# Branch order and one-by-one turns in a fused attention, router and gated-product kernel

## The chip, the cores and the metric

The kernel runs on one core of a Trainium2 chip. The metric is the device time of one execution in microseconds. The core's engines run their own instruction streams and meet through semaphores: TensorE (PE, matrix products and transposes), VectorE (DVE), ScalarE (ACT), GpSimd (POOL) and SyncE (SP, which here only issues transfers).

## The reference

Three stages, each feeding the next, all in float32:

```
scores = q k^T / sqrt(64)                  # batch 2, 8 heads, 768 positions, head size 64
keep = (key < n_sink) | (0 <= query - key < window)      # n_sink 4, window 128
x = softmax(where(keep, scores, -1e9)) v   # laid out as 1536 tokens x 512

P = exp(x w_gate - max)                    # 1536 x 8 experts, then 8 rounds of row and column scaling
y = sum over e of P[:, e] * relu(x w1[e]) w2[e]          # 512 -> 1024 -> 512, 8 experts

out = ((y w_a) * (y w_b)) w_out            # 512 -> 1536 -> 512
```

`n_sink` and `window` are inputs, so the program must also be right for other values.

## The kernel before, in words

Every float32 operand is split into a high part, which is what TensorE's reduced float32 format keeps, and a low part, the rest. A product is made of three passes: high by high, high by low, low by high. ScalarE makes high parts (a copy that rounds), VectorE makes low parts (original minus high part).

**Two ways through attention.** VectorE reads the two sizes and writes a flag, `in_range`, at the start. Each engine loads it (`chosen`, line 205) and branches. With `fits == 1` (at most 16 sinks, window at most 129) a fast path runs that computes only the needed band of the scores, for pairs of heads, with `LEAD = 2` pairs in flight. With `fits == 0` a general path runs, written with loops. With the inputs here the fast path is taken. GpSimd and TensorE have the code of the general path ahead of that of the fast path, as two Ifs after each other (TensorE: `pe.If(fits == 0)` at line 730, then `pe.If(fits == 1)`). SP, ScalarE and VectorE have an If for the fast path and an Else for the general one, so there the fast path's code stands first and a branch at its end (lines 348, 1080, 1472) passes over the general path. What follows is common to both.

VectorE's fast path starts with `in_window` (lines 1283, 1285), the low parts of queries and keys of pair 0 (`split_pair_lo`, lines 1307, 1310), `make_mask` (1291, 1294) and `mask_scores` (1321). TensorE's scores of pair 0 (line 562) wait for these low parts. At the end of attention VectorE copies the router's logits (`logits_out`, line 1419) and splits the first expert's weights (line 1385), for whose second half GpSimd forms sums (lines 430 to 435) and ScalarE high parts (line 988).

**Experts.** A product of two 2 x 2 blocked matrices is done with seven block products, P1 to P7, instead of eight. Each is six matmuls of 128 x 384 (lines 655 to 657). `sub` 0 and 1 are the two halves of the hidden columns, `pi` 0 and 1 the two batches of tokens. Sums and differences of blocks that the method needs are made by GpSimd, ScalarE (`keep`) and VectorE (`add`).

**The hand-over to the last stage.** The sum over experts (`acc`) is in token order and must be turned so that the model dimension lies on partitions. `turn_sums(v)`, v = 0 to 23, does one piece: two or four transposes on TensorE (line 726) into one PSUM bank. `x2_hi(v)` (line 1140) takes the high part on ScalarE and `x2_lo(v)` (line 1625) the low part on VectorE. Turns 0 to 11 are for batch 0, 12 to 23 for batch 1. The pieces of batch 1 alternate between two PSUM banks: turn v waits for low part v - 2. Turns 12 to 23 stand between the products of the last stage's first group (k = 0), which uses batch 0 only. The tables `LEAD_TURNS` and `FIRST_TURNS` say behind which product each turn stands. The first product of the second group (P1, k = 1, sub 0) waits until all 24 low parts exist.

The order on each engine is the order in which the code is written. On ScalarE and VectorE the parts stand between the copies and additions of group k = 0: `keep_a`, `keep_b` (ScalarE, lines 1186, 1190), `add_a`, `add_b` (VectorE, lines 1714, 1721), `gated` (VectorE, lines 1729, 1733: product of the two factors), `gated_hi` (ScalarE, 1197), `gated_lo` (VectorE, 1741), and `wo_hi`, `wo_lo`, the parts of the output weights (1202, 1747).

Of the kernel before, what the change touches and what calls it, by code (L numbers as in the profile page):

```python
# [33 lines left out]
def build(nc, qT, kT, v, sizes, w_gate, w1, w2, w_a, w_b, w_out, out):  # L34
    B, H, D, S = qT.shape
# [5 lines left out]
    KC = DM // P  # L41
# [14 lines left out]
    LEAD = 2  # L56
    RING = 4
    PAIRS = HEADS // 2
# [19 lines left out]
    with ctx:  # L78
# [95 lines left out]
        s = {n: sem(n) for n in names}  # L174
# [118 lines left out]
        def _(sp):  # L293
# [10 lines left out]
            def load_values(b):  # L304

                sp.dma_start(vs[:, b], v_rows[b][:, :, 0:P]).then_inc(s[f"v_in{b}"], 16)
                sp.wait_ge(s["sink_zero"], 1)
                sp.dma_start(vz[0:SINK, b], v_rows[b][0:SINK, 0, 0:P]).then_inc(s[f"v_in{b}"], 16)

            def load_w1(e, hf, sub):  # L310
                f0 = hf * FM * P + sub * SUBF
                sp.dma_start(raw1[:, sub], w1_rows[:, bass.ds(e * KC, KC), f0:f0 + SUBF])\
                    .then_inc(s[f"raw1_in{sub}"], 16)
# [31 lines left out]
            load_values(0)  # L345
            sp.dma_start(wg[:], w_gate.rearrange("(c p) e -> p c e", p=P)).then_inc(s["gate_in"], 16)
            fits = chosen(sp)
            with sp.If(fits == 1):
                load_values(1)
                for sub in range(2):  # L350
                    load_w1(0, 0, sub)
                for i in range(1, KC):
                    for b in range(B):
                        load_pair(i, b)
                sp.wait_ge(s["qk_lo"], 2 * PAIRS)
                load_w2(0, 0)
            with sp.Else():
                for landed in ("qk_in0", "qk_in1"):
                    sp.wait_ge(s[landed], 32)
                sp.wait_ge(s["v_in0"], 32)  # L360
                for sub in range(2):
                    load_w1(0, 0, sub)
                with sp.Fori(0, QT) as j:
                    with sp.Fori(0, KC) as c:
                        for b in range(B):
                            general_loads(j, c, b)
                sp.wait_ge(s["d_lo"], 2 * GROUPS + 2)
                load_w2(0, 0)
            load_step(0, 1)
            with sp.Fori(1, E) as e:  # L370
# [172 lines left out]
        def _(pe):  # L543
# [385 lines left out]
                        mm.then_inc(s["z_ps"], 1)  # L929

            FULL = ("P1", "P5", "P2", "P6", "P3", "P7")
            LEAD_TURNS = {"P1": (12,), "P5": (13,), "P2": (14,), "P6": (15, 16), "P3": (17,), "P7": (18,)}
            FIRST_TURNS = {"P1": (19,), "P5": (20,), "P2": (21,), "P6": (22, 23)}
            for name in FULL:
                gated_product(name, 0, 0)
                for v in LEAD_TURNS[name]:
                    turn_sums(v)
            for k in range(KT):
                for name in FULL:
                    gated_product(name, 1, k)  # L940
                    if k == 0:
                        for v in FIRST_TURNS.get(name, ()):
                            turn_sums(v)
                    if k == 0 and name == "P1":
                        gated_product("P4", 0, 0)
                if k + 1 < KT:
                    gated_product("P1", 0, k + 1)
                    gated_product("P4", 1, k)
                    for name in FULL[1:]:
                        gated_product(name, 0, k + 1)  # L950
                    project2(k, 0)
                    gated_product("P4", 0, k + 1)
                    for tt in range(1, HTILES):
                        project2(k, tt)
# [8 lines left out]
        def _(act):  # L963
# [113 lines left out]
                                     accum_out=esum[:, 0, 0:1]).then_inc(s["d_exped"], 1)  # L1077

            fits = chosen(act)
            with act.If(fits == 1):  # L1080
                for p in range(LEAD):
                    split_pair_hi(p)
                for p in range(-LEAD, PAIRS):
                    if p == -1:
                        gate_parts_hi()
                    pair(p)
            with act.Else():
                with act.Fori(0, QT) as j:
                    with act.Fori(0, KC) as c:
                        for b in range(B):  # L1090
                            for a in range(2):
                                general_head(j, c, b, a)
                act.wait_ge(s["d_t"], 1)
                nc.scalar.copy(xoh_op[:, 4, :], x32_op[:, 5, :]).then_inc(s["d_thi"], 1)
                act.wait_ge(s["d_t"], 5)
                nc.scalar.copy(xoh_op[:, 0:2, :], x32_op[:, 0:2, :])
                nc.scalar.copy(xoh_op[:, 3, :], x32_op[:, 3, :])
                nc.scalar.copy(xoh_op[:, 2, 0:BEFORE_LAST], x32_op[:, 2, 0:BEFORE_LAST])
                nc.scalar.copy(xoh_op[:, 5:7, 0:BEFORE_LAST], x32_op[:, 5:7, 0:BEFORE_LAST])\
                    .then_inc(s["d_thi"], 1)  # L1100
                act.sem_inc(s["t_hi"], 10)
                gate_parts_hi()
                ws_hi(0, 0, (0, 1, 2))

            def gate_exp():

# [100 lines left out]
            x2_hi(13)  # L1207
            x2_hi(14)
            keep_a("P6", 0, 1)
            for v in (15, 16, 17, 18):  # L1210
                x2_hi(v)
            for k in range(KT):
                first = k == 0
                keep_b("P1", k, 0)
                if first:
                    x2_hi(19)
                    keep_a("P4", 0, 3)
                keep_b("P5", k, 2)
                if first:
                    x2_hi(20)  # L1220
                    x2_hi(21)
                keep_b("P6", k, 1)
                if first:
                    x2_hi(22)
                    x2_hi(23)
                    wo_hi(0)
                gated_hi(k, 0)
                gated_hi(k, 1)
                if k + 1 < KT:
                    keep_a("P1", k + 1, 0)  # L1230
# [17 lines left out]
        def _(dve):  # L1248
# [220 lines left out]
                nc.vector.tensor_copy(x32_flat[rows, bass.ds(at, P)], ps[rows, O_BANK, 0:P]).then_inc(s["d_lo"], 1)  # L1469

            fits = chosen(dve)
            with dve.If(fits == 1):
                in_window()
                split_pair_lo(0)
                make_mask()
                mask_scores(0, (0, 1))
                split_pair_lo(1)
                for p in range(-LEAD, PAIRS):
                    if p == -1:
                        gate_parts_lo()  # L1480
                    pair(p)
            with dve.Else():
                dve.wait_ge(s["d_pos"], 2)
                for jh in range(2):
                    with dve.Fori(0, QT // 2) as j3:
# [31 lines left out]
                dve.sem_inc(s["x_ready"], 1)  # L1517
                gate_parts_lo()
                ws_lo(0, 0, (0, 1, 2))


            links = 0
# [240 lines left out]
            x2_lo(12)  # L1763
            x2_lo(13)
            add_a(0, 0)
            for v in (14, 15, 16):
                x2_lo(v)
            add_a(0, 1)
            x2_lo(17)
            add_a(0, 2)  # L1770
            for v in (18, 19, 20):
                x2_lo(v)
            for k in range(KT):
                t = k // B
                add_b(k, 0)
                if k == 0:
                    x2_lo(21)
                gated(k, 0)
                if k > 0:
                    gated_lo(k, 0)  # L1780
                if k == 0:
                    x2_lo(22)
                    x2_lo(23)
                add_b(k, 1)
                add_b(k, 2)
                gated(k, 1)
                gated(k, 2)
                if k == 0:
                    wo_lo(0)
# [56 lines left out]
```

## Time and profile before

| | |
|---|---|
| time, median of 3 runs | 1434.7 us (1434.7 to 1436.05) |
| profiled execution | 1434.7 us, its span 1432.9 us |
| TensorE busy | 1399.3 us, 98% of the span |
| VectorE, ScalarE, GpSimd busy | 55%, 35%, 14% |
| matmuls | 7592 |
| mean granted TensorE clock | 0.999 of full speed |

Times inside the execution are counted from the start of the span. Attention with its pairs ends at about 126 us, the experts at about 1149 us, the last stage fills the rest. In the answers, a name such as `ps<-xoh,wsh` reads: written tile, then the tiles read. `xoh`, `xol` are high and low parts of the tokens, `wsh`, `wsl` those of weights, `pr` the masked scores, `pt` the turned probabilities (early on also the mask's raw material), `st` and `ab` staged block products, `hh` and `hl` parts of the hidden values. A time in brackets at a row's end is how long the engine was idle before the row, and whose instruction ended that.

### The profile page before, as it was taken

Reading aid. Unit: us, or ns where it says so; the run is one execution under the profiler, and the core shown is the slowest. Engines: PE = TensorE matmul, PEld = TensorE weight load, DVE = VectorE, ACT = ScalarE, POOL = GpSimd, SP = SyncE. Lnnn points to the kernel's source line nnn. Section 1 sums busy time; section 2 is a strip of 40 time slices with the busy share of each in tenths; the row PEclk is TensorE's granted clock in tenths of the full one; section 3 lists DMA queues with packets and bytes.
Section 4 is the critical chain, followed back from the end, with each engine's and each line's share of the span. In section 5 each row is a group of like instructions: output and inputs, shape, how many; then the busy total and the mean of one; then the engine's idle time right before and its main releaser. Section 6 shows DMA issues by size and latency. Waiting matters only on the chain.

```text
span 1432.9 us, 21020 instructions
## 1 busy us (share of the span) xinstructions
PE 1399.3 (98%) x7592; PEld 1255.9 (88%) x7592; DVE 788.4 (55%) x1507; ACT 497.7 (35%) x1081; POOL 207.2 (14%) x263
## 2 busy tenths in 40 slices
PE   5988999999999999999999999999999999999999
PEld 4777889888899988889998888999888999999998
DVE  6887665544445454444545444454544566656665
ACT  5885132322223232222323222242322343232331
POOL 1256010101101010110101011010101321111100
PEclk9999999999999999999999999999999999999999
DMA  4221000101000010100001010000101001101002
GB/s 149 94 87 31 30 30 30 40 22 58 31 29 29 29 37 23 57 29 29 29 29 41 21 55 29 29 29 29 44 22 38 16 31 44 30 31 45 30 1 88
DMA packets 49726, 56.48 MB, mean 39 GB/s; under 512 B 2432, under 2 KB 37376, under 8 KB 49664
## 3 DMA queue, kind: packets, MB, share of 16 engines
q1 hardware_dynamic: 44768, 53.26, 11.5%
q10 hardware_dynamic: 4896, 2.41, 0.6%
q8 instruction: 38, 0.62, 0.2%
q14 instruction: 24, 0.20, 0.0%
HBM read 52.51 MB, written 3.15 MB: 39 GB/s over the span
## 4 chain that ended last, share of the span: by engine, by line
PE 91%; DVE 4%; ACT 4%; issue 1%; POOL 0%; DMA 0%; DVEq 0%; POOLq 0%
PE ps L655 29%; PE ps L657 29%; PE ps L656 29%; ACT pr L1007 2%; ACT pt L1016 1%; PE ps L726 1%; PE ps L585 1%; PE ps L562 0%; DVE wide L1349 0%; DVE wsl L1385 0%; DVE pr L1321 0%; DVE acc L1760 0%; DVE x L1353 0%; DVE w2l L1310 0%; PE ps L681 0%
## 5 line engine op out<-in xcount | busy, mean ns | idle before, releaser
L655 PE MATMUL ps<-xoh,wsh 128*128 128x384 f32 x1232 | 414.3, 336 | 3.0 <-ACT st L1122 3.0
L657 PE MATMUL ps<-xol,wsh 128*128 128x384 f32 x1232 | 413.2, 335 | 0.0
L656 PE MATMUL ps<-xoh,wsl 128*128 128x384 f32 x1232 | 412.7, 335 | 0.0
L655 PE MATMUL ps<-w2h,hh 128*128 128x512 f32 x912 | 360.7, 396 | 0.8 <-DVE acc L1603 0.8
L657 PE MATMUL ps<-w2l,hh 128*128 128x512 f32 x912 | 359.8, 395 | 0.0
L656 PE MATMUL ps<-w2h,hl 128*128 128x512 f32 x912 | 359.6, 394 | 0.0
L1608 DVE SCALAR_TENSOR_TENSOR acc<-ps,g_now,acc 128x512 f32<-128x512 f32 x180 | 135.1, 751 | 201.6 <-PE ps L657 201.6
L655 PEld LDWEIGHTS ps<-xoh,wsh 128*128 128x128 f32 x1232 | 231.9, 188 | 7.1 <-ACT st L1122 3.3
L656 PEld LDWEIGHTS ps<-xoh,wsl 128*128 128x128 f32 x1232 | 231.9, 188 | 3.7
L657 PEld LDWEIGHTS ps<-xol,wsh 128*128 128x128 f32 x1232 | 231.6, 188 | 0.0
L657 PEld LDWEIGHTS ps<-w2l,hh 128*128 128x128 f32 x912 | 171.7, 188 | 39.8
L655 PEld LDWEIGHTS ps<-w2h,hh 128*128 128x128 f32 x912 | 171.9, 188 | 37.0 <-DVE acc L1603 1.2
L656 PEld LDWEIGHTS ps<-w2h,hl 128*128 128x128 f32 x912 | 171.8, 188 | 35.7
L430 POOL TENSOR_TENSOR sst<-raw 128x256 f32<-128x256 f32 x44 | 32.9, 749 | 1029.5 <-DVE wsl L1385 1029.5
L1122 ACT COPY st<-ps 128x384 f32<-128x384 f32 x96 | 46.0, 480 | 374.3 <-PE ps L657 374.3
L1581 DVE TENSOR_TENSOR st<-ps,st 128x384 f32<-128x384 f32 x96 | 53.5, 558 | 124.1 <-PE ps L657 124.1
L1581 DVE TENSOR_TENSOR ab<-ps,ab 128x384 f32<-128x384 f32 x96 | 53.5, 558 | 85.7 <-PE ps L657 85.7
L1589 DVE SCALAR_TENSOR_TENSOR hl<-ps,hh 128x384 fp32r<-128x384 f32 x64 | 35.7, 558 | 77.4 <-ACT hh L1135 76.7
L988 ACT CAST wsh<-raw 128x512 fp32r<-128x512 f32 x88 | 52.1, 621 | 58.2 <-POOL raw L432 58.2
L1385 DVE TENSOR_TENSOR wsl<-raw,wsh 128x512 fp32r<-128x512 f32 x88 | 62.3, 722 | 17.9 <-ACT wsh L988 17.9
L1135 ACT ACTIVATE hh<-ps 128x384 fp32r<-128x384 f32 x64 | 31.5, 493 | 106.1 <-PE ps L657 106.1
L1122 ACT COPY ab<-ps 128x384 f32<-128x384 f32 x96 | 46.1, 480 | 55.5 <-PE ps L657 55.5
(148 smaller groups left out, 1308.5 us busy)
## 6 DMA issues: line engine op xcount, KB each, us to landing
raw<-in_w_dram SPq DMA_DIRECT2D x32, 512.0 KB, 3.5
raw<-in_w_dram SPq DMA_DIRECT2D x16, 1024.0 KB, 5.1
rk<-in_k_dram SPq DMA_DIRECT2D x8, 384.0 KB, 3.7
rq<-in_q_dram SPq DMA_DIRECT2D x8, 384.0 KB, 4.2
raw<-in_w_a_dram SPq DMA_DIRECT2D x6, 512.0 KB, 3.6
raw<-in_w_b_dram SPq DMA_DIRECT2D x6, 512.0 KB, 3.5
raw<-in_w_out_dram SPq DMA_DIRECT2D x6, 512.0 KB, 3.6
out_dram<-acc SPq DMA_DIRECT2D x12, 256.0 KB, 2.0
```

What stands on the lines that cost most here:

```text
L430: nc.gpsimd.tensor_tensor(s1, a21, a22, ALU.add).then_inc(s["s_sum"], 1)
L655: nc.tensor.matmul(o, ah, bh, start=first, stop=False, skip_group_check=True)
L656: nc.tensor.matmul(o, al, bh, start=False, stop=False, skip_group_check=True)
L657: return nc.tensor.matmul(o, ah, bl, start=False, stop=last, skip_group_check=True)
L988: nc.scalar.copy(ws_piece(wsh, sub, j), ws_raw(sub, j)).then_inc(s["w_hi"], 1)
L1007: nc.scalar.activation(t, t, ACT.Exp, bias=nmin[:, r, j:j + 1], scale=-1.0, accum_out=esum[:, r, j:j + 1]).then_inc(s["exped"], 1)
L1122: nc.scalar.copy((st, ab)[sub][:, slot, :], ps[:, bank_of(sub, name), 0:HT]).then_inc(s["kept"], 1)
L1135: nc.scalar.activation(hh[:, 2 * sub + 1, 0, :], ps[:, bank_of(sub, "P4"), 0:HT], ACT.Relu)\
L1385: nc.vector.tensor_tensor(ws_piece(wsl, sub, j), ws_raw(sub, j), ws_piece(wsh, sub, j).bitcast(F32), ALU.subtract)\
L1581: nc.vector.tensor_tensor(t, ps[:, bank_of(sub, name), 0:HT], t, ALU.add).then_inc(s["c_add"], 1)
L1589: nc.vector.scalar_tensor_tensor(out=hl[:, 2 * sub + m, half, :], in0=src, scalar=0.0, in1=hh[:, 2 * sub + m, half, :].bitcast(F32), op0=A ...
L1608: ins = nc.vector.scalar_tensor_tensor(out=acc[:, tile, :], in0=ps[:, Y_BANK + k % 2, :], scalar=g_now[:, tile:tile + 1], in1=acc[:, tile, ...
```

## The change

Three engines (SP, ScalarE, VectorE) get the layout that TensorE and GpSimd have: the general path's code first, under `If(fits == 0)`, then the fast path's under `If(fits == 1)`. The statements in each path are the same. And the 12 turns of batch 1 are spread one behind each product: 12 to 17 behind the six products of sub 0, 18 to 23 behind the six of sub 1, instead of by the two tables, with ScalarE's and VectorE's orders adapted.

```diff
@@ SP, and in the same way ScalarE (line 1080) and VectorE (line 1472)
             fits = chosen(sp)
-            with sp.If(fits == 1):
-                load_values(1)
-                for sub in range(2):
-                    load_w1(0, 0, sub)
...
-            with sp.Else():
+            with sp.If(fits == 0):
                 for landed in ("qk_in0", "qk_in1"):
                     sp.wait_ge(s[landed], 32)
...
                 sp.wait_ge(s["d_lo"], 2 * GROUPS + 2)
+                load_w2(0, 0)
+
+            with sp.If(fits == 1):
+                load_values(1)
+                for sub in range(2):
+                    load_w1(0, 0, sub)
...
@@ TensorE
-            LEAD_TURNS = {"P1": (12,), "P5": (13,), "P2": (14,), "P6": (15, 16), "P3": (17,), "P7": (18,)}
-            FIRST_TURNS = {"P1": (19,), "P5": (20,), "P2": (21,), "P6": (22, 23)}
-            for name in FULL:
+            for x, name in enumerate(FULL):
                 gated_product(name, 0, 0)
-                for v in LEAD_TURNS[name]:
-                    turn_sums(v)
+                turn_sums(12 + x)
             for k in range(KT):
-                for name in FULL:
+                for x, name in enumerate(FULL):
                     gated_product(name, 1, k)
                     if k == 0:
-                        for v in FIRST_TURNS.get(name, ()):
-                            turn_sums(v)
-                    if k == 0 and name == "P1":
+                        turn_sums(18 + x)
+                    if k == 0 and x == 0:
                         gated_product("P4", 0, 0)
@@ ScalarE
-            for v in (15, 16, 17, 18):
+            for v in (15, 16, 17):
                 x2_hi(v)
...
                 if first:
-                    x2_hi(19)
+                    x2_hi(18)
                     keep_a("P4", 0, 3)
                 keep_b("P5", k, 2)
                 if first:
+                    x2_hi(19)
                     x2_hi(20)
+                keep_b("P6", k, 1)
+                if first:
                     x2_hi(21)
-                keep_b("P6", k, 1)
+                    wo_hi(0)
+                gated_hi(k, 0)
                 if first:
                     x2_hi(22)
                     x2_hi(23)
-                    wo_hi(0)
-                gated_hi(k, 0)
                 gated_hi(k, 1)
@@ VectorE
-            for v in (14, 15, 16):
-                x2_lo(v)
+            x2_lo(14)
+            x2_lo(15)
             add_a(0, 1)
-            x2_lo(17)
+            x2_lo(16)
             add_a(0, 2)
-            for v in (18, 19, 20):
+            for v in (17, 18, 19, 20):
                 x2_lo(v)
...
                 add_b(k, 0)
-                if k == 0:
-                    x2_lo(21)
                 gated(k, 0)
...
                 if k == 0:
+                    x2_lo(21)
                     x2_lo(22)
+                add_b(k, 1)
+                gated(k, 1)
+                if k == 0:
                     x2_lo(23)
-                add_b(k, 1)
                 add_b(k, 2)
-                gated(k, 1)
                 gated(k, 2)
```

**VectorE behind the test of the flag.** Before, the rows behind the test are those of the fast path:

```order
L205 TENSOR_LOAD in_range
L205 ISA x2
L1472 COMPARE_AND_BRANCH
L1283 TENSOR_SCALAR pt<-pt,lim 128x672
L1285 SCALAR_TENSOR_TENSOR pt<-pt 128x672
L1307 TENSOR_TENSOR wsl<-rq,wsh 128x768
```

After, the general path stands behind the test, and the fast path 280 rows further on; this is where the two meet (L1511 is the second If's test):

```order
L1385 TENSOR_TENSOR wsl<-raw,wsh 128x512 x2
L1385 TENSOR_TENSOR wsl<-sst,wsh 128x768
L1472 UNCONDITIONAL_BRANCH
L1511 COMPARE_AND_BRANCH
L1283 TENSOR_SCALAR pt<-pt,lim 128x672
L1285 SCALAR_TENSOR_TENSOR pt<-pt 128x672
```

The branch over the general path has moved from the end of the fast path to its start.

**VectorE at the end of the fast path.** Before, what stands behind the last sums of attention is a branch and the general path:

```order
L1364 TENSOR_TENSOR x<-x 128x384
L1367 TENSOR_TENSOR x<-x 128x384
L1369 TENSOR_TENSOR x<-x 128x384
L1472 UNCONDITIONAL_BRANCH
L1485 UNCONDITIONAL_BRANCH
```

After, it is the common part (L1419 copies the logits):

```order
L1364 TENSOR_TENSOR x<-x 128x384
L1367 TENSOR_TENSOR x<-x 128x384
L1369 TENSOR_TENSOR x<-x 128x384
L1511 UNCONDITIONAL_BRANCH
L1419 COPY lt<-ps 40x384 x2
```

Nothing stands between the two parts any more but a branch to the next instruction.

**VectorE at the last turns.** L1625 (L1626 after) are the low parts, `st<-ps,st` is `add_b`, `st<-st,ab` is `gated`, `w2l<-raw,w2h` are the output weights. Before:

```order
L1721 TENSOR_TENSOR st<-ps,st 128x384
L1625 TENSOR_TENSOR xol<-ps,xoh 128x2x128
L1729 TENSOR_TENSOR st<-st,ab 128x384
L1625 TENSOR_TENSOR xol<-ps,xoh 128x4x128 x2
L1721 TENSOR_TENSOR st<-ps,st 128x384 x2
L1729 TENSOR_TENSOR st<-st,ab 128x384 x2
L1747 TENSOR_TENSOR w2l<-raw,w2h 128x512 x2
```

After:

```order
L1722 TENSOR_TENSOR st<-ps,st 128x384
L1730 TENSOR_TENSOR st<-st,ab 128x384
L1626 TENSOR_TENSOR xol<-ps,xoh 128x2x128
L1626 TENSOR_TENSOR xol<-ps,xoh 128x4x128
L1722 TENSOR_TENSOR st<-ps,st 128x384
L1730 TENSOR_TENSOR st<-st,ab 128x384
L1626 TENSOR_TENSOR xol<-ps,xoh 128x4x128
L1722 TENSOR_TENSOR st<-ps,st 128x384
L1730 TENSOR_TENSOR st<-st,ab 128x384
L1748 TENSOR_TENSOR w2l<-raw,w2h 128x512 x2
```

The last low part now has an addition and a product between it and the one before it. On TensorE turn 23 (four transposes) stands behind P7, directly ahead of the second group's first product, where before turns 22 and 23 stood together behind P6. On ScalarE the two casts of the output weights and the first gated cast now stand ahead of the last two high parts.

## Rows read from the trace of the kernel before

**Rows 1.** The page, chain that ended last: shares of the span by engine.
```profile
PE 91%; DVE 4%; ACT 4%; issue 1%; POOL 0%; DMA 0%; DVEq 0%; POOLq 0%
```

**Rows 2.** Branch instructions by line: ns min/median/max, first and last start in us.
```profile
L730 PEldq COMPARE_BRANCH  x1: 5486/5486/5486, 5.9 to 5.9; - x1
...
L1472 DVEq COMPARE_BRANCH x2: 50/56/63, 5.8 to 125.4; - x2
```

**Rows 3.** Chain of waits, 4 to 14 us: start, us, what.
```profile
5.94 0.58 DVE pt L1283
...
9.23 2.51 issue
11.74 1.71 PE ps L562 x12
13.45 0.43 DVE pr L1321
```

**Rows 4.** Timeline at the end of attention, VectorE, then TensorE: start, us, instruction, idle.
```profile
125.81 0.55 DVE L1369 TENSOR_TENSOR x<-x 128x384 f32<-128x384 f32 x1
128.43 1.01 DVE L1419 COPY lt<-ps 40x384 f32<-40x384 f32 x2 [2.07 <-PE ps L681]
...
125.38 0.33 PE L681 MATMUL ps<-xol,wgs 128*128 128x384 f32 x1
```

**Rows 5.** Chain of waits, 125 to 134 us.
```profile
127.48 1.01 POOL xol L446
...
133.90 0.44 PE ps L655
```

**Rows 6.** GpSimd's line 432: ns min/median/max, first and last start.
```profile
L432 POOL TENSOR_TENSOR raw<-raw x44: 725/742/1388, 113.4 to 1366.6; 128x256 f32<-128x256 f32 x44
```

**Rows 7.** Stretches: us, busy PE, PEld, DVE, ACT, POOL, clock, DMA share, GB/s.
```profile
5.90:11.40 5.50, 0.00 (x0) 0.00 (x0) 4.58 (x6) 3.26 (x4) 1.18 (x2) 1.00 0.94 274
125.40:128.40 3.00, 3.00 (x19) 3.00 (x18) 0.96 (x2) 1.77 (x3) 1.89 (x2) 1.00 0.15 52
```

**Rows 8.** Timeline of VectorE, the mask's last step.
```profile
10.08 0.51 DVE L1294 TENSOR_SCALAR mask<-pt 128x672 f32<-128x672 f32 x1
```

**Rows 9.** Chain of waits, 1149 to 1168 us: turns 15 and 16, 20, 22 and 23.
```profile
1154.69 1.00 PE ps L726 x8
...
1162.06 0.44 PE ps L726 x4
...
1164.83 0.87 PE ps L726 x8
```

**Rows 10.** Timeline of TensorE: first matmul of the second group.
```profile
1167.62 0.33 PE L655 MATMUL ps<-xoh,wsh 128*128 128x384 f32 x1
```

**Rows 11.** Timeline of ScalarE, the last turns.
```profile
1164.86 0.48 ACT L1190 COPY st<-ps 128x384 f32<-128x384 f32 x1 [0.69 <-PE ps L657]
1165.30 1.08 ACT L1140 CAST xoh<-ps 128x512 fp32r<-128x512 f32 x2
1166.26 1.15 ACT L1202 CAST w2h<-raw 128x512 fp32r<-128x512 f32 x2
1167.30 0.52 ACT L1197 CAST hh<-st 128x384 fp32r<-128x384 f32 x1
```

**Rows 12.** Timeline of VectorE, the last turns.
```profile
1165.92 1.29 DVE L1625 TENSOR_TENSOR xol<-ps,xoh 128x512 fp32r<-128x512 f32 x2 [0.82 <-ACT xoh L1140]
1167.12 1.25 DVE L1721 TENSOR_TENSOR st<-ps,st 128x384 f32<-128x384 f32 x2
1168.30 1.02 DVE L1729 TENSOR_TENSOR st<-st,ab 128x384 f32<-128x384 f32 x2
```

**Rows 13.** Stretches, TensorE alone: us, busy, granted clock, DMA share, GB/s.
```profile
14.94:18.35 3.41, 1.92 (x16) 1.00 0.75 249
...
131.00:134.40 3.40, 0.50 (x3) 1.00 0.00 0
134.40:137.80 3.40, 3.40 (x12) 0.50 0.38 126
```

More of the change, by code:

```diff
@@ L347, in _ @@
             fits = chosen(sp)
-            with sp.If(fits == 1):
-                load_values(1)
-                for sub in range(2):
-                    load_w1(0, 0, sub)
[L352 to L356, printed above, removed]
-            with sp.Else():
+            with sp.If(fits == 0):
                 for landed in ("qk_in0", "qk_in1"):
@@ L367, in _ @@
                 sp.wait_ge(s["d_lo"], 2 * GROUPS + 2)
+                load_w2(0, 0)
[3 more added lines that the diff above has]
+                    load_w1(0, 0, sub)
+                for i in range(1, KC):
+                    for b in range(B):
+                        load_pair(i, b)
+                sp.wait_ge(s["qk_lo"], 2 * PAIRS)
                 load_w2(0, 0)
@@ L1079, in _ @@
             fits = chosen(act)
[L1080 to L1087, printed above, removed]
+            with act.If(fits == 0):
                 with act.Fori(0, QT) as j:
@@ L1103, in _ @@
                 ws_hi(0, 0, (0, 1, 2))
+            with act.If(fits == 1):
+                for p in range(LEAD):
+                    split_pair_hi(p)
+                for p in range(-LEAD, PAIRS):
+                    if p == -1:
+                        gate_parts_hi()
+                    pair(p)
             def gate_exp():
@@ L1471, in _ @@
             fits = chosen(dve)
[L1472 to L1482, printed above, removed]
+            with dve.If(fits == 0):
                 dve.wait_ge(s["d_pos"], 2)
@@ L1519, in _ @@
                 ws_lo(0, 0, (0, 1, 2))
+            with dve.If(fits == 1):
+                in_window()
+                split_pair_lo(0)
+                make_mask()
+                mask_scores(0, (0, 1))
+                split_pair_lo(1)
+                for p in range(-LEAD, PAIRS):
+                    if p == -1:
+                        gate_parts_lo()
+                    pair(p)
             links = 0
```

## The prediction

> **What bounds the kernel now.** Start with the page's chain of waits: 91% of the span is TensorE, ScalarE and VectorE have 4% each, no transfer has a part [rows 1]. So nearly all the time is matmuls that follow each other with no gap, and the change adds and removes no arithmetic. What can move is time at places where TensorE stands still, or where a step ahead of the matmul stream sits on the chain. I therefore read three short stretches: the start (0 to 14 us), where the If is taken; the end of attention (125 to 134 us), where the branch over the general path stands now; and the stretch 1149 to 1168 us with the 12 second-half turns.
>
> At the start the reader is to see that a branch is not free. All engines test the flag near 5.9 us. VectorE's test takes 50 to 63 ns and it goes on with the next instruction. TensorE, whose program already has the general path first, spends 5486 ns in the same instruction [rows 2]. It comes back at 11.39 us and starts its first matmul at 11.74, though the operands were ready when VectorE finished at 9.23: the chain shows 2.51 us of "issue" there [rows 3]. So VectorE has about 2.5 us of cover behind TensorE's own stall, and from 11.74 on the chain runs through all three engines without a transfer, so a late start is carried to the end of attention.
>
> **Part 1, the general path put first (SP, ScalarE, VectorE).** Only VectorE's general path is long: some 280 rows of its order, against about two dozen each on ScalarE and SP. Before, VectorE jumps over it once, at the end of attention; now once, at 5.9 us, over the same rows.
>
> What the jump costs at its old place: VectorE finished its sum at 126.36 (125.81 plus 0.55), and the first of the two logits tiles that it copies next was complete at 125.71 (the eighth of its matmuls, 125.38 plus 0.33), yet it started at 128.43, after 2.07 us idle [rows 4]. From the branch at 125.4 that is 3.0 us. ScalarE's branch at the same time delayed nothing visible.
>
> What its removal there gives: nothing. The chain leaves VectorE at 126.4 and goes over GpSimd (127.48, the split of the last outputs, then the weight sums) to ScalarE and reaches TensorE at 133.90 [rows 5]. VectorE's copies and splits of weights are ready well before. GpSimd's step takes 1.39 us once where its median is 0.74 [rows 6], with a VectorE split beside it; with VectorE 2 us earlier that collision falls on the GpSimd step before it instead. Bounds: minus 0.65 (no collision) to plus 0.65 (one more); I take 0.
>
> What the jump costs at its new place is not in the trace, so I bound it. From below: 3.0 us from branch to first work, as at 125.4, when the DMA engines were 15% busy. From above: TensorE's 5.49 us, at the very moment of the new jump, with the DMA engines 94% busy by the first loads [rows 2, 7]. The nearest row is TensorE's, same time and same load; I take 5.3 us, so VectorE starts its first mask step at 11.1 instead of 5.94: 5.2 us later. It then needs its 3.3 us (5.94 to 9.23) to the low parts, done at 14.4, and the mask, before ready at 10.59 (10.08 plus 0.51 [rows 8]), is ready at 15.8. TensorE would start at 14.5 and have the first two tiles' scores (1.71) when they are wanted, so VectorE itself is the bound: tile 0's two scores, with half the columns of tile 1's 0.43 and 0.35, take about 0.4 (an estimate), and tile 1 starts at 16.2 where it started at 13.45 [rows 3, 8]. Loss: 5.2 - 2.4 = **2.8 us**. By the lower bound (2.9 us later) it is 2.9 - 2.4 = 0.5. With no stall it is 0. Loads do not care: SP's next load of keys waits for the low parts of pair 0 and slips to 14.4, but those keys belong to pair 2, which is split only after pair 1's scores are masked.
>
> The Trainium skill (Runtime: NRT & Kernel Launch, Instruction fetch mechanics) says that a taken branch out of a two-page window of instructions stalls for a fetch, and gives a page as 256 instructions. The 5486 ns of TensorE and the 2.07 us of VectorE agree with the stall. By its size of window VectorE's target at the start would be held already and cost 0, which would make the sum 1436.8; the 2.07 us after a jump over the same rows speak against that.
>
> **Part 2, the turns one by one.** Each turn v must go TensorE, then ScalarE's high part, then VectorE's low part. The products of the next group may start only when all 24 low parts exist. Before, turns 22 and 23 stand two products (2.1 us) ahead of that product: the low parts end at 1167.21 (1165.92 plus 1.29) and the product starts at 1167.62, 0.4 us of slack [rows 10, 12]. Now turn 23 is the last thing before it, so its whole way is bare, and the ways through ScalarE and VectorE have got longer too.
>
> TensorE's side: on the chain a turn of four transposes costs 0.44 with the hand-over to the product behind it, the two double turns cost 1.00 and 0.87 [rows 9]. As four single turns they cost 1.76: 0.11 less. A product is six matmuls of 0.17, 1.04. So TensorE could begin the next group's product at 1167.5. Counted back over turn 23 (0.44), a product (1.04), turn 22 (0.44), a product (1.04) and turn 21 (two transposes, 0.22), product P6 ends at 1164.3.
>
> ScalarE's side, now in this order: keep P6, high part 21, the two output weight casts, the first gated cast, high part 22. A row here starts about 0.1 before the shown end of the one ahead (1166.26 plus 1.15 against 1167.30), so they count 0.44, 0.3 (half the columns of the 0.6 of a full part, an estimate), 1.04, 0.42 and 0.6; from a product's end to its keep I take 0.2. 1164.3 + 0.2 + 0.44 + 0.3 + 1.04 + 0.42 + 0.6 = 1167.3 [rows 11]. Before, the weight casts and the gated cast came after part 23. High part 23 can start when turn 23 has drained, 0.3 after its 1167.4, and is done at 1168.3.
>
> VectorE's side: low part 22 at 1167.35 (0.60), add (0.55), product of the gates (0.55, which waits for the add), low part 23 (0.69, so that the two make 1.29): 1167.35 + 0.60 + 0.55 + 0.55 + 0.69 = 1169.7 [rows 12]. It is ready to take part 23 only at 1169.0, later than ScalarE's 1168.3, so the order on VectorE ends the wait. TensorE starts at 1169.7 instead of 1167.62: **2.1 us**. Bounds: bare latency without VectorE's queue, 1168.3 + 0.69 = 1169.0, is 1.4; with every start 0.1 later it is 2.5. The lead half has no such join: turns 14 to 17 are each wanted a product and more later than their low parts exist. Behind the join the next wait of TensorE is for the gates' low parts, seven products on, which moves along. Nothing later takes the time back: the matmul stream is solid to the end.
>
> **Sum.** The profiled execution took 1434.7 us (span 1432.9 and 1.8 around it), which is also the median of the three runs, so it needs no correction. 1434.7 + 2.8 + 0 + 2.1 = **1439.6 us**. About 0.2%, 2.9 us, is what a measurement of this kernel can tell from no change; this is 4.9.
>
> **Rivals.**
> 1. Short stall: VectorE's fetch is served as fast as at 125.4, and TensorE's cover swallows most. For: the 3.0 us are of the same engine and the same jump. Against: the DMA engines are 94% busy instead of 15%. 1434.7 + 0.5 + 2.1 = 1437.3.
> 2. No stall at the start: the target is held. For: at that time little has been executed, ScalarE and SP see none. Against: the same jump did stall later. 1434.7 + 2.1 = 1436.8.
> 3. The clock. After a wait of TensorE of 3 us (131.0 to 134.4 holds 0.50 us of work) the granted clock was 0.50, its 1.2 GHz level, for 3.4 us, with 12 matmuls where 20 of 0.17 fit; after a half-idle stretch at 14.94 (1.92 of 3.41 busy) it stayed at 1.00 [rows 13]. The new gap at the join is 2.2 us, between the two. If it tips the clock, 8 matmuls of 0.17 us are lost: +1.4, 1441.0.
> The skill (TensorE: Matmul & The Clock Gate) says that an idle stretch brings the slow level; that agrees with 0.50 at 134.4.
> 4. The other side, one mechanism: at 133.9 TensorE really waits for work behind VectorE's stall, and the profile credits ScalarE wrongly. Then 2.07 us go, and TensorE's shorter wait no longer lowers the clock, which returns 1.4. It decides if VectorE's chain is the last to end there. If the start stall is covered as well: 1434.7 - 2.1 - 1.4 + 2.1 = 1433.3. Against: the chain names GpSimd and then ScalarE [rows 5].
>
> **How the numbers follow.** Forecast 0.50 (its own range 1438.6 to 1440.6), short stall 0.18, none 0.10, clock 0.12, other side 0.05, remainder 0.05. Half of the short-stall case, with a stall somewhat over 3.0, passes 1437.6 and counts as slower. Slower: 0.50 + 0.12 + 0.09 + 0.01 = 0.72; same: 0.10 + 0.09 + 0.03 = 0.22; faster 0.06. The range from 1436.7 to 1441.6 takes in all but rival 4 and the tails.
>
> **What would show it.** VectorE's branch near 5.9 us lasting several microseconds, its first mask step near 11, the first matmul near 14.5 and the end of attention 2.8 us later. VectorE's copy of the logits right behind the last sum, and TensorE still waiting for ScalarE before its fourth product. A gap of about 2.2 us in TensorE ahead of the first product of the second group, put down to VectorE's low part; ScalarE's weight casts ahead of the last two high parts. It is wrong if VectorE starts near 6 us or the first matmul stays at 11.7, if the join has no gap, or if the time is under 1437.6.

## The result, and the profile after

The changed kernel takes 1442.2 us (median of 5 executions, 1440.8 to 1443.8) against 1434.7 us (median of 5, 1432.6 to 1436.05): ratio 1.0059, 95% interval 1.0048 to 1.0070. It is slower by 7.5 us by the medians and by 8.5 us by the ratio, where 4.9 us were forecast; the median lies 0.6 us above the range. Two executions far outside their kernels' others, 1732.64 us of the run "turns alone" and 7360.8 us of the kernel before on the same chip, are in no median and no ratio below. The page of the changed kernel opens with these lines:

```profile
span 1444.1 us, 21020 instructions
...
PE 1404.1 (97%) x7592; PEld 1258.3 (87%) x7592; DVE 789.1 (55%) x1507; ACT 499.1 (35%) x1081; POOL 206.0 (14%) x263
...
PE 88%; DVE 5%; ACT 5%; issue 2%; POOL 0%; DMA 0%; DVEq 0%; POOLq 0%
```

The same 7592 matmuls; TensorE's share of the chain fell from 91% [rows 1] to 88%. The profiled execution took 1445.95 us, 11.25 more than the profiled one of before, and I first account for this pair by the distance between the same matmul in both traces, called its lateness below.

**The start.** The instructions that answer to [rows 2], by line (count, minimum/median/maximum in ns, first and last start):

```profile
L731 PEldq COMPARE_BRANCH  x1: 5550/5550/5550, 5.9 to 5.9; - x1
...
L1472 DVEq COMPARE_BRANCH  x1: 67/67/67, 5.8 to 5.8; - x1
...
L1511 DVEq COMPARE_BRANCH  x1: 50/50/50, 11.6 to 11.6; - x1
```

and the chain of waits that answers to [rows 3] (start, us, what):

```profile
5.83 0.07 DVEq L1472
5.89 5.69 issue
11.58 0.05 DVEq L1511
...
11.69 0.58 DVE pt L1283
```

The first test takes 67 ns, then VectorE issues nothing for 5.69 us and stands at the second test: the stall shows not in the branch's own duration, as it does on TensorE, but in the "issue" behind it. The timeline adds TensorE's start:

```profile
11.69 0.57 DVE L1283 TENSOR_SCALAR pt<-pt,lim 128x672 f32<-128x672 f32 x1 [6.81 <-issue]
...
15.03 0.47 PE L563 MATMUL ps<-wsh,wsl 64*128 64x128 f32 x2 [15.03 <-DVE wsl L1310]
...
128.84 0.55 DVE L1369 TENSOR_TENSOR x<-x 128x384 f32<-128x384 f32 x1
129.31 0.54 DVE L1419 COPY lt<-ps 40x384 f32<-40x384 f32 x1
```

The first matmul comes 3.3 us later than before and waits for VectorE; once attention has settled its matmuls are 3.0 us late. The last two rows answer to [rows 4]: the first logits tile is copied right behind the last sum, which is 3.0 us late itself, and the 2.07 us of idle time are gone. (The second tile, at 130.87, waits 1.02 us for TensorE.)

**The end of attention.** Chain of waits, to hold against [rows 5]:

```profile
131.52 1.16 POOL sst L431
132.75 0.74 POOL raw L433
134.25 1.20 POOL sst L436
135.48 0.83 ACT wsh L985
136.31 0.39 ACT st L1120
136.74 0.69 PE ps L656
```

GpSimd and ScalarE end the wait as before, at 136.74 instead of 133.90, +2.84. Line 433 is back at 0.74 us, but line 431 ahead of it now takes 1.16: the collision with VectorE [rows 6] moved one step forward, and the two steps together take 1.90 us instead of 2.09. So of 3.0 us at the start 0.2 are given back here.

The profiled execution of before was also on the fast side at this place. Its first GpSimd step took 0.73 us; in the profiles of five experiments below that keep VectorE's old branches it took 1.97 to 2.08. Here are the rows of "gate product between the additions" (timeline: start, us, instruction):

```profile
128.69 1.99 POOL L430 TENSOR_TENSOR sst<-raw 128x256 f32<-128x256 f32 x1
130.76 0.73 POOL L432 TENSOR_TENSOR raw<-raw 128x256 f32<-128x256 f32 x1
```

In these five VectorE was idle for 1.84 to 1.95 us at its branch, instead of 2.07 (before, and VectorE's Else back, which has before's form), and TensorE's wait lasted 3.5 to 3.7 us instead of 3.0. All six profiles with VectorE's new branches have neither 2.07 us of idle time nor a slow first step (1.2 and 0.74 us, TensorE's wait 2.7 to 2.8). Against most profiles of the old layout the new one therefore gains some 0.8 us here, not 0.2. Why 0.1 to 0.2 us in VectorE's return decide between the two old forms was not tested.

Stretches (start:end, us, busy PE, PEld, DVE, ACT, POOL, clock, DMA share, GB/s), of the end of attention and of the join:

```profile
133.00:136.00 3.00, 0.96 (x6) 0.64 (x4) 0.69 (x1) 1.14 (x2) 2.92 (x4) 1.00 0.00 0
136.00:142.80 6.80, 6.06 (x19) 6.06 (x20) 3.66 (x4) 3.53 (x8) 6.20 (x6) 0.50 0.24 80
...
1171.70:1173.70 2.00, 0.01 (x1) 0.00 (x0) 1.90 (x5) 1.10 (x2) 0.00 (x0) 1.00 0.00 0
1173.70:1177.10 3.40, 3.27 (x10) 3.30 (x11) 3.15 (x6) 0.89 (x2) 0.00 (x0) 0.50 0.00 2
```

Behind the wait the granted clock is at 0.50, its 1.2 GHz level, for 6.8 us, where before it was for 3.4 [rows 13]; the matmuls behind it are 4.0 us late instead of 2.8, so that stretch cost 1.2 more.

**The join.** The chain from high part 21 to the second group's first product, beside [rows 9 to 12]:

```profile
1169.02 0.28 ACT xoh L1138
1169.30 1.04 ACT w2h L1200 x2
1170.33 0.41 ACT hh L1195
1170.74 0.50 ACT xoh L1138
1171.30 0.57 issue
1171.87 0.56 DVE st L1722
1172.62 0.38 issue
1173.00 0.69 DVE xol L1626
1173.83 0.66 PE ps L656
```

The product starts at 1173.83 where it started at 1167.62: the lateness goes from 4.0 to 6.2, 2.2 us more. TensorE does nothing from 1171.7 to 1173.7 (second pair of stretches above), the last low part (L1626 at 1173.00) ends the wait, and behind it the clock is at 0.50 again for 3.4 us: then the lateness is 7.8, 1.6 us more.

**Every later group.** Here lies what the forecast has no term for. From the first product of one group to that of the next, before took 22.96 us and after takes 23.3, ten times in a row from the second group behind the join on. Before, the timeline of one such group shows (start, us, instruction):

```profile
1190.10 1.24 DVE L1721 TENSOR_TENSOR st<-ps,st 128x384 f32<-128x384 f32 x2
1191.25 1.02 DVE L1729 TENSOR_TENSOR st<-st,ab 128x384 f32<-128x384 f32 x2
...
1191.62 0.33 PE L655 MATMUL ps<-xoh,wsh 128*128 128x384 f32 x1
```

and after:

```profile
1197.92 0.55 DVE L1722 TENSOR_TENSOR st<-ps,st 128x384 f32<-128x384 f32 x1
1198.58 0.56 DVE L1730 TENSOR_TENSOR st<-st,ab 128x384 f32<-128x384 f32 x1
1199.05 0.55 DVE L1722 TENSOR_TENSOR st<-ps,st 128x384 f32<-128x384 f32 x1
...
1199.66 0.44 PE L656 MATMUL ps<-xoh,wsh 128*128 128x384 f32 x1
```

The diff moves the product of the gates, `gated(k, 1)`, between `add_b(k, 1)` and `add_b(k, 2)` for every k, not for k = 0 alone. TensorE's product P4 waits for the second addition (the later of the two rows of L1721, or of L1722), which reads the bank that P4 writes. Before, both additions were done at 1191.34 and P4 began at 1191.62, 0.28 us later, and that slack is the same in all ten groups; now the second ends at 1199.60 and P4 begins at 1199.66, behind it. The waits between 1185 and 1420 us (engine, tile, line, what it waits for; us in total, times, longest) name the pair, which has no row in the same view of before:

```profile
PEld ps L656 <- DVE st L1722: 3.7, 10, 0.4
```

These are ten waits of 0.37 us. By the distance between the same matmuls, the time they cost is 0.34 us a group, 3.4 in all (the lateness goes from 7.8 to 11.3). With it the account of the profiled pair closes: 2.8 (start and end of attention) + 1.2 (clock in attention) + 2.2 (join) + 1.6 (clock behind it) + 3.4 (groups) = 11.2, against 11.25 measured. Without the two clock terms it is 8.4, near the 8.5 of the ratio. The profiled execution had more time at the lower clock than most: its mean granted clock is 0.996, and the 21 others run from 1440.5 us at 1.000 to 1445.3 at 0.996.

### The profile page after: what moved, and what is told of

The parts are those of the page before. It is cut to its first block, busy times and chain, and to the rows that moved or that the text cites. A ratio compares the mean times of both kernels' runs of the same rounds, so it can differ in the third digit from the quotient of the medians.

```text
span 1444.1 us, 21020 instructions
## 1 busy us (share of the span) xinstructions
PE 1404.1 (97%) x7592; PEld 1258.3 (87%) x7592; DVE 789.1 (55%) x1507; ACT 499.1 (35%) x1081; POOL 206.0 (14%) x263
## 3 DMA queue, kind: packets, MB, share of 16 engines
q1 hardware_dynamic: 44768, 53.26, 11.4%
## 4 chain that ended last, share of the span: by engine, by line
PE 88%; DVE 5%; ACT 5%; issue 2%; POOL 0%; DMA 0%; DVEq 0%; POOLq 0%
PE ps L656 29%; PE ps L658 28%; PE ps L657 28%; ACT pr L1004 2%; DVE st L1722 1%; ACT pt L1013 1%; PE ps L727 1%; DVE wide L1349 0%; PE ps L586 0%; ACT st L1188 0%; DVE pr L1321 0%; ACT hh L1195 0%; DVE wsl L1385 0%; DVE acc L1761 0%; DVE x L1353 0%
```

## The experiments

Medians are given with the number of executions, ratios against the kernel before on the same chip with their 95% intervals. "One execution" is a single profiled one; it can tell a step in the trace, not a microsecond of the total.

**Loop back.** The changed kernel, with the order of additions of before for all k > 0.

```diff
                 add_b(k, 1)
+                if k > 0:
+                    add_b(k, 2)
                 gated(k, 1)
                 if k == 0:
                     x2_lo(23)
-                add_b(k, 2)
+                    add_b(k, 2)
                 gated(k, 2)
```

> The changed kernel with one thing put back: in the groups k > 0 VectorE does both additions (add_b 1 and 2) ahead of the gate product, as before; the first group k = 0 keeps the new order. Theory A (the moved gate product delays TensorE's P4 by about 0.33 us in each of 11 groups): the distance from group to group in the last stage returns from 23.3 to 22.95 us and the time falls by 3.6 us against the changed kernel, to about 1438.6. Theory B (the time above the forecast is the slower TensorE clock after the gaps): the distance stays at 23.3 and the time at 1442. Theory C (a code fetch or a changed operand place slows the last stage): stays at 23.3 too.

1438.96 us (11), ratio 1.0026 (1.0018 to 1.0035). A group is 22.96 us long again, the wait for L1722 is gone from the view of the waits, and start and join stay as in the changed kernel. The chain of its join:

```profile
1171.98 0.69 DVE xol L1626
1172.81 0.41 PE ps L656
```

Two lines moved back are worth 3.3 us by the medians (4.7 by the two ratios), 3.4 by the groups in the traces.

**Turns alone.** The kernel before with the orders of turns, parts and additions of after, the branches untouched.

```diff
-                for v in LEAD_TURNS[name]:
-                    turn_sums(v)
+                turn_sums(12 + x)
... (and the orders on ScalarE and VectorE as in the change)
```

> Only the turns and their orders on TensorE, ScalarE and VectorE are changed, the branches are those of before. Theory A: no loss at the start, a gap of 2.1 us at the first product of the second group, and 11 x 0.33 = 3.6 us in the groups: 1434 + 5.7 = about 1440, plus 1.4 where the clock falls after the gap. Theory B: 1434 + 2.1, plus up to 3 of clock, at most 1439, groups of 22.95 us.

1440.97 us (5), ratio 1.0041 (1.0028 to 1.0054), by which it is +5.9 us: the step at the join is 2.2 again, a group 23.3, VectorE starts at 5.92. In the trace the turns' half of the diff costs 2.2 + 3.4 = 5.6 us.

**Layout alone.** The other half.

```diff
-            with dve.If(fits == 1):
-                in_window()
...
-            with dve.Else():
+            with dve.If(fits == 0):
...
+            with dve.If(fits == 1):
+                in_window()
... (SP and ScalarE in the same way)
```

> Only the branches are changed on SP, ScalarE and VectorE; turns as before. Theory A: VectorE's first step after the test at 11.7 us, attention ends 3.0 us later, groups of 22.95 us: 1434 + 3.0 = 1437. Theory B, that the new layout slows more than the start (more fetches in the last stage): above 1438 and groups over 22.95.

1437.62 us (11), ratio 1.0017 (1.0008 to 1.0026), by which it is +2.4 us. VectorE's first mask step is at 11.53 and the first matmul at 14.87, no gap at the join, groups of 22.96. By their ratios the two halves give 5.9 + 2.4 = 8.3; together they measured 8.5.

**VectorE's Else back.** The changed kernel with VectorE alone in the old layout (SP and ScalarE keep the new).

```diff
-            with dve.If(fits == 0):
+            with dve.If(fits == 1):
+                in_window()
...
+            with dve.Else():
                 dve.wait_ge(s["d_pos"], 2)
```

> The changed kernel with VectorE's If and Else put back as before; SP and ScalarE keep the new layout. Theory A: all of the loss at the start is VectorE's, so its first step is at 5.9 us, the first matmul at 11.7, and the time 3.0 below the changed kernel, about 1439.3. Rival: part of the loss comes from SP's or ScalarE's jump, then the first matmul stays later than 11.7 or the end of attention keeps some of the 3 us.

1441.44 us (5), ratio 1.0047 (1.0034 to 1.0060). VectorE starts at 5.93 and the first matmul at 11.58, as before; join and groups stay as after. In the trace the whole cost of the start belongs to VectorE; SP's and ScalarE's layout costs nothing. The total missed its expectation: 1441.44 us is 0.8 below the changed kernel where 3.0 were expected. It is +6.7 us by the ratio (4.9 to 8.6), which holds the 5.9 of the turns but is too wide to price the start by itself. The clock explains the miss as far as the record goes: the five executions have a mean granted clock of 0.996 to 0.999, the changed kernel's five 0.998 to 1.000, and the difference of the two averages, 0.0018 of 1440 us, is 2.6 us (an estimate).

**Short general path.** Layout alone, with VectorE's general path cut to about thirty instructions. It leaves out the loops over the heads, so it holds for sizes of the fast path only.

```diff
             with dve.If(fits == 0):
-                dve.wait_ge(s["d_pos"], 2)
-                for jh in range(2):
-                    with dve.Fori(0, QT // 2) as j3:
...
+                dve.sem_inc(s["d_lo"], 2 * GROUPS)
```

> As the kernel with only the branches changed, but VectorE's general path leaves out its loops over heads, so that the new jump passes over some 30 instructions instead of some 300; with other sizes its output would be wrong, the fast path is whole. Theory A (the stall is the fetch of code that lies far off): VectorE reaches the second test at about 5.9 us and its first step at 6.0, TensorE's branch still takes 5.3 to 6.4 us and its first matmul is back near 11.7. Rival (any taken branch, or the wait for the flag, costs this at that time): second test still near 11.5.

One execution, 1435.15 us. VectorE's first step (timeline: start, us, instruction, idle time before it) and the first matmul:

```profile
6.14 0.65 DVE L1285 TENSOR_SCALAR pt<-pt,lim 128x672 f32<-128x672 f32 x1 [1.26 <-issue]
...
12.46 0.48 PE L563 MATMUL ps<-wsh,wsl 64*128 64x128 f32 x2 [12.46 <-issue]
```

The same branch, taken over 30 instructions, costs 0.2 us (6.14 for 5.94): distance decides, not the two Ifs. The first matmul at 12.46 is TensorE's own stall, which was 6.21 us here; over all profiles with that stall and the loads as before it was 5.3 to 6.4.

**Late loads.** Layout alone, with SP's loads of pair 1, the first values and the gate weights issued after the flag is read.

```diff
             load_pair(0, 0)
+            fits = chosen(sp)
             load_pair(0, 1)
...
-            fits = chosen(sp)
```

> As the kernel with only the branches changed, but SP issues the loads of pair 1, of the first values and of the gate weights after the test of the flag instead of before, so the DMA engines have little left to do at 5.9 us. Theory A (the length of the stall, 5.7 us against 3.0 at the end of attention, is the queue of loads ahead of the fetch): VectorE's stall falls to 3 to 4 us, TensorE's branch from 5.3 to 6.4 us to 3.5 to 4.5. Rival (the fetch of the fast path's first code always takes 5.5 us, the end of attention is quicker for another reason): both stay at 5.5 or more.

One execution, 1435.96 us.

```profile
8.80 0.57 DVE L1285 TENSOR_SCALAR pt<-pt,lim 128x672 f32<-128x672 f32 x1 [3.92 <-issue]
```

The same jump, 2.7 us shorter: VectorE stood 2.8 us instead of 5.5 in layout alone, TensorE 3.39 instead of 6.1. With fewer loads queued, both stalls are about half as long. That fits the prediction's choice: the price at the quiet end of attention, 3.0 us, was the lower bound and TensorE's at the busy start the right neighbour.

**TensorE's fast path first.** The kernel before, with TensorE in an If for the fast path and an Else for the general one: the reverse of what the change did to VectorE.

```diff
-            with pe.If(fits == 0):
-                for jh in range(2):
...
             with pe.If(fits == 1):
...
+            with pe.Else():
+                for jh in range(2):
```

> The kernel before, with TensorE too having the fast path first and the general one in an Else. Theory A (the 2.5 us ahead of the first matmul are TensorE's code fetch, and at the end of attention TensorE has 3.0 us of idle time that can hide its jump): first matmul at 9.4 us instead of 11.7, the end of attention 2.4 us earlier, logits matmuls up to 3 us late behind the last weigh, TensorE's wait for ScalarE shorter by as much, time 1434.8 - 2.4 = 1432.4. Rival: the jump at the end of attention is on the path, then the gain is given back: 1434.8.

1434.11 us (11), ratio 0.9989 (0.9980 to 0.9998). The first matmul comes at 9.31, 2.4 us earlier. But the jump at the end of attention is now TensorE's, and it has no cover (chain of waits):

```profile
120.59 0.88 DVE wide L1348
121.47 4.64 issue
126.12 5.05 PE ps L681 x20
```

4.64 us of "issue" ahead of the logits' matmuls, which end up later than before (124.07) though everything ahead was earlier, and the granted clock is at 0.50 from 125.6 to 129.0. TensorE's first product behind attention then starts 0.2 us later than before, so all of the 2.4 us are handed back there. The total is still 1.5 us lower, because the 3.4 us at the lower clock that before follow this wait [rows 13] now fall ahead of it, on the logits' matmuls. So the expectation's 1432.4 failed, and the rival had the mechanism right.

**Low part 23 first.** Turns one by one, loops as before, and for k = 0 the last low part ahead of the additions.

```diff
                 if k == 0:
+                    x2_lo(21)
                     x2_lo(22)
                     x2_lo(23)
                 add_b(k, 1)
                 add_b(k, 2)
```

> Branches as before, turns one by one, VectorE's additions in the groups k > 0 as before, and in the first group low part 23 ahead of both additions and the gate product. Theory A (VectorE's order ends the wait at the second group's first product): the step from the last transpose to that product falls from 2.4 us to about 1.7. Rival (the bare way of turn 23 through both engines): stays at 2.4. In both, groups of 22.96 us.

One execution, 1437.5 us. From the last transpose's start to the product: 1.77 us, from 2.39 in turns alone.

```profile
1168.88 0.60 ACT xoh L1136
1169.50 0.70 DVE xol L1623
1170.34 0.41 PE ps L655
```

High part, low part, product with no VectorE step between: of the 2.2 us, 0.6 were VectorE's queue and 1.6 are the bare way, which the forecast put at 1.4.

**High parts first.** The same, with ScalarE's last two high parts also ahead of the weight casts.

```diff
                 if first:
+                    x2_hi(21)
                     x2_hi(22)
                     x2_hi(23)
                     wo_hi(0)
```

> As the kernel with low part 23 ahead of VectorE's additions, and besides on ScalarE the high parts 22 and 23 ahead of the output weight casts and the gate cast. Theory A (after VectorE's order only the bare way of turn 23 is left): the step to the second group's first product stays at 1.8 us, since ScalarE already was free when the turn had drained. Rival (ScalarE's casts still hold up part 23): it falls to 1.3 us or less.

One execution, 1435.24 us; the step is 1.76. ScalarE's order was worth nothing: the way from drained bank through both engines is what a turn directly ahead of its consumer costs. (This execution had no stretch at the lower clock in attention, which is 1.6 of the 2.3 us by which its total is lower.)

**Gate product between the additions.** The kernel before, with nothing but the missed edit.

```diff
                 add_b(k, 1)
-                add_b(k, 2)
+                if k == 0:
+                    add_b(k, 2)
                 gated(k, 1)
+                if k > 0:
+                    add_b(k, 2)
                 gated(k, 2)
```

> The kernel before with the changed kernel's order of two VectorE instructions alone: in the groups k > 0 of the last stage the gate product 1 stands between the additions 1 and 2. Theory A: each group 23.30 us instead of 22.96, the time 11 x 0.35 = 3.8 us longer than before, 1438.6, with nothing else moved. Rival (the longer groups need the one-by-one turns too): 22.96 and 1434.8.

1439.55 us (7), ratio 1.0027 (1.0016 to 1.0038), +3.9 us. Its waits in the stretch of above:

```profile
PEld ps L655 <- DVE st L1721: 3.7, 10, 0.4
```

The same row as in the changed kernel, with no change anywhere else: ten groups of 23.3 us, 3.4 us in the trace. This is the largest single term of the result.

**TensorE's general path rolled.** The kernel before; TensorE's general path is written as a loop with four heads of code instead of sixteen.

```diff
             with pe.If(fits == 0):
-                for jh in range(2):
-                    with pe.Fori(0, QT // 2) as j3:
-                        for kh in range(2):
-                            with pe.Fori(0, 2) as kk:
...
+                with pe.Fori(0, QT) as j:
+                    with pe.Fori(0, KC) as c:
```

> The kernel before, with TensorE's general path written as one double loop over query tiles and head pairs, so that it holds 4 heads of code instead of 16; its statements and the fast path are the same, and only the fast path is run here. Theory A (a branch stalls when its target lies beyond the code that is held): TensorE's branch falls from 5.5 us to about 0.1, first matmul at 9.3 us, no stall at the end of attention either, attention ends 2.4 us earlier: 1434.8 - 2.4 = 1432.4, a ratio of 0.9983. Rival (the stall belongs to the first fetch, whatever the distance): branch over 5 us, time as before.

1432.7 us (11), ratio 0.9977 (0.9968 to 0.9986): faster than the kernel before, by 2.9 us by the medians. The branch (ns, start in us):

```profile
L730 PEldq COMPARE_BRANCH  x1: 375/375/375, 5.9 to 5.9; - x1
```

0.375 us instead of 5.49, the first matmul at 9.69, and the matmuls of attention 2.2 us earlier. No engine has a long jump at the end of attention but VectorE. The trace shows GpSimd's slow first step there (1.99 us), and behind attention 1.9 of the 2.2 us are left, against the profiled execution of before, which had the fast step.

**Changed kernel, TensorE's path rolled.** The same loop in the changed kernel.

> The changed kernel with TensorE's short general path of the rolled loop. Theory A (VectorE's fetch alone sets the start, TensorE's stall was cover): TensorE's branch takes 0.1 us, the first matmul stays near 15.0 us unless VectorE's fetch is served sooner without TensorE's beside it. Rival (the two fetches delay each other): VectorE's second test clearly earlier than 11.4.

One execution, 1442.7 us. Its start on the chain:

```profile
5.63 0.07 DVEq L1470
5.70 5.16 issue
10.86 0.05 DVEq L1509
```

TensorE's branch took 0.37 us, yet the first matmul came at 14.3, where the changed kernel's came at 15.0: TensorE's stall was mostly cover beside VectorE's. VectorE's second test came at 10.86 instead of 11.4 to 11.8, so the expectation's rival, that the two stalls lengthen each other, is not excluded. One execution can't tell a shorter stall from chance: VectorE's stall was 5.2 us here and 5.5 to 5.9 in the three other profiles with this jump and the loads as before.

## Why the prediction was too low

- **Start, +2.8.** Right in place and cause, and near in size. The stall was 5.7 us for 5.3, the first mask step at 11.69 for 11.1, the first matmul at 15.03 for 14.5, and attention 3.0 us late for 2.8. Its working also held: TensorE's own stall was cover of about 2.5 us, and VectorE itself was the bound. Late loads and short general path show both sides: 2.8 us when less is queued, 0.2 when the distance is short. Rivals 1 and 2 fall with that. With rival 2 falls the estimate from the Trainium skill (Runtime: NRT & Kernel Launch, Instruction fetch mechanics) that its window of two pages of 256 instructions holds VectorE's target, some 280 rows on: here VectorE stalled 5.7 us, so the target was not held.
- **End of attention, 0.** Right in the path, inside the bounds of 0.65 either way for the profiled pair, but not nothing: VectorE's 2.07 us went, GpSimd and ScalarE still end the wait, and the collision moved and cost 0.2 less, 0.8 less than in most profiles of the old layout. That the first two terms sum to 2.84 where 2.8 was forecast is partly luck: 3.0 less 0.2. Rival 4 had this wait on VectorE, and falls.
- **Join, +2.1.** Measured 2.2, with VectorE's order as the last wait, inside the bounds of 1.4 to 2.5. Of these, 1.6 are the bare way and 0.6 the addition and the gate product ahead of the last low part.
- **"Nothing later takes the time back: the matmul stream is solid to the end."** This is the step that failed. Under part 2 the change was followed through group k = 0 alone; the moved addition stands in the loop's body and is issued in every group. The stream was solid only because the second addition ended 0.28 us ahead of the product that needs its bank, and the move used that up and 0.34 us a group more, 3.4 in all, shown by taking it out (loop back) and by making it alone (gate product between). With that term the sum would have been 2.8 + 2.1 + 3.4 = 8.3, 1443.0 us, inside the interval of the ratio.
- **The clock, rival 3.** Partly seen. Behind the gap of 2.1 us at the join the clock fell in the profile of the changed kernel and cost 1.6 us (1.4 had been worked out), but not in those of loop back, turns alone, VectorE's Else back and the changed kernel with the rolled path, which have the same gap. It is a chance in each execution and not a term of the median.

What stays open is small: loop back measured 3.7 us over before (2.6 to 5.0) where start, end of attention and join give 5.0 in the traces. The profile of before was on the fast side at the end of attention; with the 0.6 us that five other profiles of the old layout lose there, it would be 4.4 (an estimate). How much of the rest is a different share of executions with a stretch at the lower clock was not settled.

## What to carry to other kernels

A moved statement in a loop is priced once for each iteration: go through every trip of the loop for the buffer that the moved instruction frees, and read from the trace the slack between its end and its next user (here 0.28 us, and a step of 0.56 was put ahead of it). A branch over unused code is free only while its target is near; put the unused path where the engine has nothing to do, make it short by rolling its loops, or let it fall beside another engine's stall, and count what is left uncovered. The last piece that a consumer waits for wants a product or two of distance from it: here 1.6 us of bare way against 1.04 for a product.

## What the runs showed of the hardware

- A taken branch over a long path stalled by distance and by load: VectorE over some 280 rows 5.2 to 5.9 us with the first loads queued and 2.8 with fewer, over about 30 instructions 0.2; TensorE 5.3 to 6.4 us over sixteen heads of code at the start, 3.4 there with fewer loads queued, 4.4 at 121.5 us, 0.375 over four heads.
- On VectorE the stall did not lengthen the branch's own row (67 ns); it stands as "issue" behind it. On TensorE it is in the branch's row (5550 ns).
- GpSimd's sum of 128x256 (L430) took 0.73, 1.2 or 2.0 us at the end of attention, with VectorE's copies and splits beside it at different moments; its median over the kernel is 0.74.
- The same gap of 2.1 us in TensorE was followed by the clock at 0.50 in one of five profiles; the wait at the end of attention by 3.4 us of it in the kernel before, 6.8 in the changed one, none in layout alone and in "high parts first". The 22 executions of the changed kernel spread by 5.4 us, from 1440.5 at a mean granted clock of 1.000 to 1445.95 at 0.996.
